# A fused attention and two-MLP kernel on one core: the last tile of the second MLP gets a body of its own

## The reference

```python
def _moe_ref(x, w_in, w_out):                      # first MLP
    h = x @ w_in                                   # 384 -> 2048
    return np.maximum(0.01 * h, h) @ w_out         # 2048 -> 384

def _moe2_ref(x, expert_emb, tau, w1, w2):         # second MLP
    ...
    expert_idx = np.argmax(logits, axis=1)
    ...
    for e in range(E):
        mask = expert_idx == e
        h = np.maximum(x[mask] @ w1[e], 0.0)       # 384 -> 1024
        out[mask] = gate_w[mask, None] * (h @ w2[e])   # 1024 -> 384
```

## Time and profile before

| | |
|---|---|
| median of 3 runs | 835.08 us (834.29 to 836.28) |
| the profiled execution | 834.27 us |
| its span, first to last instruction | 832.3 us |
| PE busy | 814.6 us (98%) |
| DVE, ACT, POOL busy | 564.4, 438.8, 203.3 us |
| granted TensorE clock | 0.999 |

### The profile page before, as it was taken

One profiled execution on the slowest core, in us unless ns is written; L12 is line 12 of the kernel. 1 busy time (PEld: TensorE's weight loads), 2 busy tenths in 40 slices (PEclk: granted clock), 3 DMA queues, 4 the chain that ended last, 5 costly groups with the idle time before them and its releaser, 6 DMA issues.

```text
span 832.3 us, 18049 instructions
## 1 busy us (share of the span) xinstructions
PE 814.6 (98%) x5633; PEld 763.7 (92%) x5633; DVE 564.4 (68%) x1315; ACT 438.8 (53%) x924; POOL 203.3 (24%) x286
## 2 busy tenths in 40 slices
PE   6999999999999999999999999999999999999997
PEld 6899999999999999999999999999889998898896
DVE  6879788879889878879888855635452512545463
ACT  6675564464464465465456435553552533565563
POOL 5611111122103013103113001303343323334433
PEclk9999999999999999999999999999999999999999
DMA  9975432155242141232210001414531513376392
GB/s 215 206 150 130 77 68 39 34 92 69 51 73 34 31 84 33 39 83 38 39 34 30 1 16 30 171 47 128 168 124 40 185 47 100 134 259 201 92 315 66
DMA packets 165307, 78.56 MB, mean 94 GB/s; under 512 B 135486, under 2 KB 153253, under 8 KB 165090
## 3 DMA queue, kind: packets, MB, share of 16 engines
q1 hardware_dynamic: 156402, 64.81, 32.3%
q0 software_dynamic: 4544, 10.85, 4.0%
q10 hardware_dynamic: 4272, 1.82, 0.9%
HBM read 112.90 MB, written 11.63 MB: 150 GB/s over the span
## 4 chain that ended last, share of the span: by engine, by line
PE 85%; SPq 7%; DVE 3%; issue 2%; ACT 1%; DMA 1%; POOL 0%; DVEq 0%; ACTq 0%; POOLq 0%
PE bank L1065 22%; PE bank L1044 21%; PE bank L1117 13%; PE bank L1153 13%; SPq L458 3%; PE bank L1134 3%; PE bank L970 2%; PE bank L937 2%; PE bank L998 2%; PE bank L993 2%; SPq L483 1%; PE bank L1099 1%; PE bank L978 1%; SPq L471 1%; SPq L490 1%
## 5 line engine op out<-in xcount | busy, mean ns | idle before, releaser
L1044 PE MATMUL bank<-xhl,WRh 128*128 128x384 f32 x768 | 219.0, 339 | 0.7 <-DVE WRl L1715 0.5
L1044 PEld LDWEIGHTS bank<-xhl,WRh 128*128 128x128 f32 x768 | 141.3, 188 | 1.2 <-issue 1.2
L1411 ACT COPY gw<-bank 128x384 f32<-128x384 f32 x128 | 61.6, 481 | 152.3 <-PE bank L1044 150.9
L1065 PE MATMUL bank<-WRh,gh 128*128 128x384 f32 x384 | 135.8, 354 | 0.0
L1044 PE MATMUL bank<-xhl,WRl 128*128 128x384 f32 x384 | 130.0, 339 | 0.0
L1065 PE MATMUL bank<-WRh,gl 128*128 128x384 f32 x384 | 129.8, 338 | 0.0
L1065 PE MATMUL bank<-WRl,gh 128*128 128x384 f32 x384 | 129.7, 338 | 0.0
L1734 DVE TENSOR_TENSOR gl<-gw,gh 128x384 fp32r<-128x384 f32 x128 | 72.2, 564 | 56.6 <-ACT gh L1417 52.7
L1417 ACT CAST gh<-gw 128x384 fp32r<-128x384 f32 x128 | 65.2, 510 | 76.7 <-DVE gw L1727 64.4
L1727 DVE SCALAR_TENSOR_TENSOR gw<-gw 128x384 f32<-128x384 f32 x128 | 75.7, 592 | 31.3 <-ACT gw L1411 30.9
L1902 DVE TENSOR_TENSOR hl<-bank,hh 128x512 fp32r<-128x512 f32 x56 | 36.1, 686 | 84.0 <-ACT hh L1452 83.7
(11 more groups left out here) (199 smaller groups left out, 1639.7 us busy)
## 6 DMA issues: line engine op xcount, KB each, us to landing
stage<-in_moe_w_dram SPq DMA_DIRECT2D x96, 768.0 KB
Kn<-in_k_dram SPq DMA_DIRECT2D x24, 192.0 KB, 3.4
Vn<-in_v_dram SPq DMA_DIRECT2D x24, 192.0 KB, 3.2
x_moe<-x2s SPq DMA_DIRECT2D x24, 192.0 KB, 2.0
Rn<-in_r_dram SPq DMA_DIRECT2D x21, 192.0 KB, 2.8
wraw<-in_moe_w_out_dram SPq DMA_DIRECT2D x4, 768.0 KB, 7.4
eraw<-in_moe_w_dram SPq DMA_DIRECT2D x4, 768.0 KB, 8.9
Wn<-in_w_dram SPq DMA_DIRECT2D x152, 16.0 KB, 1.8
```

What stands on the lines that cost most here:

```text
L1044: mm = pe.matmul(bank[F_BANK[n % 2]][:, 0:GN], win(t_)[:, f // 4, k_, cols], xhl[G % 2][:, a, k_, :], start=(k_ == 0 and n_ == 0), stop=(k ...
L1065: mm = pe.matmul(bank[O_BANK[i]][:, 0:DM], a[:, z, cols], wout(t_)[:, f, :], start=(f == 0 and n_ == 0), stop=(f == FT - 1 and n_ == 2))
L1411: act.copy(gw[:, n % 2, :], bank[F_BANK[n % 2]][:, 0:GN]).then_inc(s_g0, 1)
```

## The change

`last_tiles` is kept for SP and POOL. PE, ACT and DVE get `ending_tiles` instead, which tests one tile ahead: in front of the body of tile j it asks whether there is a tile j + 1. If not, it jumps to an `Else` block that holds the last tile's body and the drain. There are ten such blocks. On PE the last tile is `features`, the first half of the result of the tile in front, `turn_h` of the last tile, and the second half of that result; then `result` of the last tile follows as before. On ACT the last tile is two `relu`, `h_hi(j, 0)`, a wait until the result of the tile in front is complete, `h_hi(j, 1)`, and only then `scaled(j - 1)`; the features' input and the weights of a next tile are left out. On DVE only the two `h_lo` stay.

```diff
+        def ending_tiles(eng, n, body, last, drain):
+            def level(j):
+                if j + 1 == MT:
+                    last(j)
+                    return drain(j + 1)
+                with eng.If(n > j + 1):
+                    body(j)
+                    level(j + 1)
+                with eng.Else():
+                    last(j)
+                    drain(j + 1)
+            with eng.If(n > NT):
+                level(NT)
+            with eng.Else():
+                drain(NT)
...
             def result(j, s_):
+                result_half(j, s_, 0)
+                result_half(j, s_, 1)
...
+            def last_tile(j):                       # PE
+                s_, half = j % 2, j // 2
+                features(j, s_, half)
+                result_half(j - 1, 1 - s_, 0)
+                turn_h(j)
+                result_half(j - 1, 1 - s_, 1)
...
-                last_tiles(pe, n_used, lambda j: tile(j, j % 2, j // 2), lambda n: result(n - 1, (n - 1) % 2))
+                ending_tiles(pe, n_used, lambda j: tile(j, j % 2, j // 2), last_tile, lambda n: result(n - 1, (n - 1) % 2))
...
+            def last_tile(j):                       # ACT
+                s_, half = j % 2, j // 2
+                relu(j, 0)
+                relu(j, 1)
+                h_hi(j, 0)
+                act.wait_ge(s_o2, j)
+                h_hi(j, 1)
+                scaled(j - 1, 1 - s_, half - 1 + s_)
...
+            def last_tile(j):                       # DVE
+                h_lo(j, 0)
+                h_lo(j, 1)
```

More of the change, by code:

```diff
@@ L1137, in result, with result_half @@
             def result(j, s_):
+                result_half(j, s_, 0)
+                result_half(j, s_, 1)
+            def result_half(j, s_, a):
                 early_ = whole(j) and j < K1
                 _, (w2h, w2l) = views(eh, el) if early_ else expert(s_)
-                if not whole(j) or j > 1:
+                if a == 0 and (not whole(j) or j > 1):
                     pe.wait_ge(s_o2e, j - 1)
[L1142 to L1155, removed]
+                pe.wait_ge(s_hhi, 2 * j + a + 1)
+                pe.wait_ge(s_hlo, 2 * j + a + 1)
+                if early_:
+                    pe.wait_ge(s_phi, a + 3)
+                    pe.wait_ge(s_plo, a + 3)
+                else:
+                    pe.wait_ge(s_ehi, 4 * (j - K1) + a + 3)
+                    pe.wait_ge(s_elo, 4 * (j - K1) + a + 3)
+                for f in range(4 * a, 4 * a + 4):
+                    for n_, (h_, w_) in enumerate(((hh, w2h), (hh, w2l), (hl, w2h))):
+                        mm = pe.matmul(bank[R_BANK[s_]][:, 0:DM], h_[:, f, :], w_[:, f, :],
+                                       start=(f == 0 and n_ == 0), stop=(f == FT2 - 1 and n_ == 2))
+                if a == 1:
+                    mm.then_inc(s_o2, 1)
+            def last_tile(j):
[4 more added lines that the diff above has]
+                result_half(j - 1, 1 - s_, 1)
             def tile(j, s_, half):
@@ L1592, in all_tiles @@
                 tiles(act, tile)
-                last_tiles(act, n_used, lambda j: tile(j, j % 2, j // 2), lambda n: scaled(n - 1, (n - 1) % 2, (n - 1) // 2))
+                ending_tiles(act, n_used, lambda j: tile(j, j % 2, j // 2), last_tile,
+                             lambda n: scaled(n - 1, (n - 1) % 2, (n - 1) // 2))
             act.wait_ge(s_flag, 1)
@@ L2037, in all_tiles @@
                 tiles(dve, tile)
-                last_tiles(dve, n_used, lambda j: tile(j, j % 2, j // 2), lambda n: None)
+                ending_tiles(dve, n_used, lambda j: tile(j, j % 2, j // 2), last_tile, lambda n: None)
             dve.wait_ge(s_flag, 1)
```

## The result

| | before | after |
|---|---|---|
| median | 834.94 us (6 runs, 833.60 to 836.28) | 839.48 us (6 runs, 837.41 to 840.96) |
| ratio, 95% interval | | 1.0055 (1.0041 to 1.0068) |
| the profiled execution, its span | 834.27, 832.3 us | 837.41, 835.7 us |
| mean granted TensorE clock | 0.999 | 0.997 |

The change costs 4.5 us (3.4 to 5.7). The profiled execution is the fastest of the six. Up to the start of tile 26's transposes it was 0.9 us ahead of the one of before (810.23 against 811.14), for no reason that the change touches (it was 0.8 us ahead already when the second MLP began), and behind that point it lost 4.3 us. The stretch from t0 to the end of the span, the tail, is 21.1 us before and 25.4 us after.

A forecast was written before the change was run, and what follows sets the result against it. PE, busy 98%, was taken to bound the kernel; with PE's jump exposed, POOL's chain starts scaled(27) at 830.55 instead of 827.45, 3.1 us later. Added to the 835.08 us median: 838.2 us, range 835.2 to 840.0.

The forecast's parts named there:

- the forecast case: Tail: PE's jump exposed and the end set by the chain through POOL; +3.1 us, chance 0.72.
- the new order: ACT: scaled(26) behind h_hi(27, 1) and the moved transposes, its start going from 821.01 to 822.46 without PE's delay.
- features late: PE, tile 27's features: delayed by the far jump standing in front of them; taken as 2.5 us.
- its sign: PE's branch in front of tile 27's features was to last 3.4 to 4.8 us in the changed kernel's profile.
- PE's gap: PE before result(27): the 1.29 us gap goes, and 0.08 us at the next matmul; gain 1.37 us.
- The covers: h_hi and h_lo of tile 27 run under 2.1 us halves of results, covered by 0.5 us or more.
- the middle of the first two: PE's jump delay: 2.5 us, between 2.1 (quiet fetch) and 2.9 us (packet slowed while the weight load lasts).
- The chain through POOL: From scaled(26) by scatter, drain and gcol to scaled(27): 5.59 us, which starts scaled(27) 3.1 us later.
- R1: PE's jump stays hidden, but POOL's chain still holds scaled(27): +0.6 us, 835.7 us; chance 0.12.
- R2: Jump hidden and POOL's drain 2.87 us or less: 0.3 to 1.3 us faster, 834.3 us; chance 0.04.
- R3: Only PE's delay counts, gcol of tile 27 not hanging on the scatter: +1.1 us, 836.2 us; chance 0.05.
- ACT's and DVE's jumps: Their moved jumps in tile 27 stay covered; both relu done by 819.8, with PE needing them at 821.2.

The follow-up runs named there:

- e1: Changed kernel, but PE's row of levels ends at tile 27, so no far jump on PE; 834.02 us, ratio 1.0005 to the kernel before.
- e12: Kernel before, but PE has no code for tiles 28 to 33, so no jump before the last result; 834.83 us, ratio 0.9997.
- e2: Changed kernel, but POOL copies the gates of tiles 24 and on in front of the previous tile's scatter; 838.92 us, ratio 1.0061 to the kernel before.
- e3: Changed kernel's test one tile ahead, but the last tile keeps the old order of PE and ACT; 838.33 us, ratio 1.0060 to the kernel before.
- e4: Changed kernel, but two of tile 27's four weight pieces are loaded in one row only; 836.17 us, ratio 1.0031 to the kernel before.
- e10: Repeat of e6, the short PE test with POOL's drain and copies before the scatter; 834.15 us, ratio 0.9991 to the kernel before.
- e7: Changed kernel with twelve unread matmuls on PE between tile 26's transposes and the test; 838.64 us, ratio 1.0042 to the kernel before.
- e5: Changed kernel without PE's far jump, and POOL's drain and copies before the previous tile's scatter from tile 24 on; 834.73 us, ratio 1.0001 to the kernel before.
- e6: Changed kernel with a short PE test behind each tile's features, and POOL's drain and copies before the scatter; 833.79 us, ratio 0.9982 to the kernel before.

## Why the prediction was right in direction and short in size

Forecast: +3.1 us, the range 835.2 to 840.0. Measured: +4.5 us, 839.48. It follows the forecast case, with a jump exposed and the end set through POOL. Point by point, in us behind t0, with the forecast's own terms:

| term of `scaled(27)`'s start | forecast | measured | from |
|---|---|---|---|
| `scaled(26)` before | 9.87 | 9.87 | |
| the new order | +1.45 | +1.38 | e1 |
| features late | +2.5 | +3.32 | after |
| slower clock | 0 | +1.39 | after |
| `scaled(26)` to `scaled(27)` | +5.59 | +5.08 | after |
| sum | 19.41 | 21.04 | |
| against 16.31 before | +3.10 | +4.73 | |

From `scaled(27)` to the end it took 4.82 us before and 4.38 after, which gives back 0.44 us: a tail of +4.3 us. That the total stayed inside the range, near its upper end, is in part luck: the way to `scaled(26)` was 2.1 us longer than forecast, and what lies behind it 0.95 us shorter, two errors of opposite sign. The branch of 5.25 us is also outside the 3.4 to 4.8 us that the prediction gave as its sign.

- **PE's gap: right.** 1.37 us forecast, 1.39 in e1. The covers held: in after there is no gap behind `turn_h(27)`. e12 shows that the gap was not the jump's.
- **The jump exposed: right; its delay: the term that was mis-sized.** The step that failed is "I take 2.5 us, the middle of the first two", from one slowed packet that the earlier trace rows showed. In after the packet itself was hardly slowed, 1.0 us (3.2% of 16 engines over the 2 us from 811 on), like the quiet one of the earlier trace rows:

```profile
q8 instruction: 1, 0.02, 3.2%
```

  What grew was the wait in front of it, from 1.0 to 2.8 us. I had priced the load on the transfer, and here it fell on the start of the transfer. The packet of the earlier trace rows was a poor guide: its 2.43 us ran on into the next load (share 0.89 from 796.5 and 1.03 from 797.0 on), while that of after moved when its load was over. Against this, the branch began 1.3 us in front of t0 and not 0.74, and gave 0.6 us back. In after, e2, e3 and e4 it starts 0.05 to 0.06 us after the end of ACT's second `relu` of tile 26, on which `turn_h(26)` waits (808.87 in after; in before 810.33, for the test at 810.4), so it is ACT that was early against t0: -1.33 + 5.25 + 0.30 = 4.22, where the forecast had -0.74 + 3.45 + 0.3 = 3.0 and 0.4 for load. The 0.3 us from the end of the branch to the first feature came out at 0.30. e4 shows the load as the cause: with two of the four weight pieces gone the same branch is 1.67 us shorter.

  Each of the six far jumps has such a packet of its own behind its start, and the short tests of e10 none that they wait for (0.31 us at most). The Trainium skill, page "Runtime: NRT & Kernel Launch", section "Instruction fetch mechanics", limits the forced fetch to taken branches that leave the pages already held. By that rule, the runs agree on both sides.

- **The clock: missing.** The forecast had no step for what an idle PE does to the work behind it. In after and e2 the granted clock fell to about half behind 3.2 and 3.5 us of idle time, in e3 it did not behind 3.2 us, and it did not in e4 (1.6 us) and e7 (0.6 us). It cost 1.4 us in after. The forecast left PE idle for over 2 us itself, and a price for the work behind that belonged into its upper end. The profiled execution of after had the clock fall once, at a mean of 0.997; two slower ones had means of 0.993 and 0.994 (840.96 and 839.49 us), but without a trace it is not shown where they lost it.
- **The chain through POOL: right in kind.** `scaled(27)` was released by `gcol`, as the one wait of the earlier trace rows had said. 5.59 us was 0.5 us too long, all from the drain (3.30, not 3.82), that is, from the landing of tile 26's scatter that it waits for (2.9 us, not 3.5). It is not the gate alone: e2 shows that the scatter of tile 27 would have been held by the drain and `si` all the same.
- **R1 (jump hidden)** was put at +0.6 us. e1 is that case, built: +0.4 us, tail +0.24. R1's mechanism, PE's gain turned into a wait for POOL, is what e1's profile shows. **R2** (-0.3 to -1.3 us) needed both a hidden jump and a short chain on POOL. e5, e6 and e10 bring both about, and their last scatters start 0.4 to 1.4 us earlier than before, or 1.4 us in all three if the late start of the features is taken off. The totals are 0, -1.5 and -0.75 us, and in the profiled executions the stretch behind SP's jump took more than the gain. **R3** (only PE's delay counts) falls with the release by `gcol`; in e3, where POOL is off the path, PE's delay counts alone, but the gap is back, and it costs as much.
- **ACT's and DVE's jumps** were covered as worked out: ACT's stood at 813.6, and its first `relu` waited for PE.
- **The tiles before** did not move: 9.6 us from `features` to `features` in both, up to tile 26 (802.59 - 793.00 and 801.68 - 792.09).

## What to carry to other kernels

A jump out of a row of written-out code held PE's sequencer for 3.3 us or more here, and up to 5.2 us when a weight load was under way. It costs what the work already in the engine's queue does not cover. Put the test where the queue holds more work than that, away from a weight load, or keep its target near. Look at the jump of the engine that ends the program in the same way: when the last output lands earlier, that jump can be what is left. Before an engine's gap is closed at the end of a kernel, follow every consumer of the results that are moved back: here all of 1.4 us turned into a wait for another engine's scatter, drain and copies. A drain behind a scatter has to be counted as the scatter's time to landing. And if PE is made idle for some microseconds, count the matmuls behind it at half clock in one bound of the sum.

## What the runs showed of the hardware that I had not expected

- The time that a load adds to an instruction fetch behind a far jump lies in front of its packet: 1.0 and 1.1 us at 0.26 and 0.14 of the DMA engines' time, 2.8 us at 1.04, and the packet moves as the load ends. The 2.3 to 2.5 us from the packet's start to the end of the branch hardly change.
- The same idle time of PE (3.2 us) was followed by half the granted clock in one execution and not in another.
- POOL's drain ends about 0.13 us after the landing of the indirect transfer in front of it. Behind the scatter of tile 26 that made it 3.3 to 5.1 us long, with no other work on POOL; this moves the end more than a swap of two ACT instructions does.
- SP's last far jump, whose record shows 38 ns, was followed by 2.7 to 3.4 us without a record in e5, e6 and e10, though the last scatter had landed by then, and this set the end of the span. In before and after the same stretch lies under the wait for that landing.
